# Low parts of the weight units and two differences moved to DVE, low part of k to POOL, the output's additions a period later

## The reference

```
scores = scale * q_c @ k_full.T
a = exp(scores - max); a = a / (sum(a) + 1e-9)
out[chunk] = a @ v_full
```

## Time and profile before

| | |
|---|---|
| three runs, median (lowest to highest) | 1243.87 us (1243.09 to 1247.61) |
| profiled execution | 1244.59 us, span 1242.8 us |
| busy, share of the span | PE 92%, weight loads 84%, DVE 72%, POOL 56%, ACT 46% |
| mean granted TensorE clock | 0.98 |
| first layer with attention | until about 740 us |
| second layer | 740 to 1242.8 us |
| DMA | 192 MB, 154 GB/s over the span |

### The profile page before, as it was taken

One profiled execution on the slowest core, in us unless ns is written; L12 is line 12 of the kernel. 1 busy time (PEld: TensorE's weight loads), 2 busy tenths in 40 slices (PEclk: granted clock), 3 DMA queues, 4 the chain that ended last, 5 costly groups with the idle time before them and its releaser, 6 DMA issues.

```text
span 1242.8 us, 19258 instructions
## 1 busy us (share of the span) xinstructions
PE 1149.0 (92%) x6624; PEld 1045.7 (84%) x6624; DVE 892.0 (72%) x1233; ACT 565.9 (46%) x1230; POOL 696.3 (56%) x542
## 2 busy tenths in 40 slices
PE   5789999999999999989999999999899999799988
PEld 4789998899889899889989997887677887588876
DVE  7778677577676666675874626568996688986678
ACT  7565555455445455454554324523425343245331
POOL 6276255555556556553652615669556675666573
PEclk9799999999999999999999999999899999899999
DMA  5244144333443443443243316655476554375545
GB/s 185 93 158 155 70 138 149 139 135 134 141 144 124 154 138 115 160 134 123 93 157 130 119 42 239 199 181 179 146 260 228 197 194 162 133 253 189 188 135 170
DMA packets 83985, 192.00 MB, mean 154 GB/s; under 512 B 5568, under 2 KB 9664, under 8 KB 83904
## 3 DMA queue, kind: packets, MB, share of 16 engines
q1 hardware_dynamic: 67008, 153.12, 36.1%
q10 hardware_dynamic: 16896, 37.75, 8.9%
HBM read 148.91 MB, written 41.94 MB: 154 GB/s over the span
## 4 chain that ended last, share of the span: by engine, by line
PE 36%; issue 22%; POOL 20%; DVE 13%; DMA 4%; ACT 4%; POOLq 0%; ACTq 0%; DVEq 0%; SPq 0%
POOL g_lo L396 5%; POOL pair_split L420 5%; PE p_y L1087 4%; PE p_y L1089 4%; PE p_y L1088 4%; DMA qkv_raw<-qkv 3%; POOL gs_lo L486 3%; POOL w_raw L415 2%; PE p_y L1077 2%; PE p_h L1061 2%; PE p_y L1078 2%; PE p_y L1079 2%; PE p_h L1062 2%; PE p_h L1063 2%; PE p_h L1087 2%
## 5 line engine op out<-in xcount | busy, mean ns | idle before, releaser
L396 POOL TENSOR_TENSOR g_lo<-g_raw,g_hi 128x384 fp32r<-128x384 f32 x112 | 120.8, 1079 | 174.1 <-ACT g_hi L572 173.3
L486 POOL TENSOR_TENSOR gs_lo<-hidden,gs_hi 128x1024 fp32r<-128x1024 f32 x60 | 161.0, 2699 | 78.7 <-ACT gs_hi L691 78.7
L1061 PE MATMUL p_h<-x_hi,w_hi 128*128 128x384 f32 x512 | 179.5, 351 | 13.2 <-DVE g_raw L825 12.0
L1077 PE MATMUL p_y<-g_hi,w_hi 128*128 128x384 f32 x512 | 176.2, 344 | 0.0
L1062 PE MATMUL p_h<-x_lo,w_hi 128*128 128x384 f32 x512 | 174.3, 340 | 0.0
L1063 PE MATMUL p_h<-x_hi,w_lo 128*128 128x384 f32 x512 | 174.2, 340 | 0.0
L572 ACT ACTIVATE g_hi<-g_raw 128x384 fp32r<-128x384 f32 x128 | 67.1, 525 | 232.6 <-DVE g_raw L825 231.9
L1079 PE MATMUL p_y<-g_hi,w_lo 128*128 128x384 f32 x512 | 171.5, 335 | 0.0
L1078 PE MATMUL p_y<-g_lo,w_hi 128*128 128x384 f32 x512 | 171.5, 335 | 0.0
L1087 PE MATMUL p_y<-gs_hi,down_ring 128*128 128x512 f32 x336 | 133.3, 397 | 12.9 <-DVE rest L932 8.6
L1088 PE MATMUL p_y<-gs_lo,down_ring 128*128 128x512 f32 x336 | 132.5, 394 | 0.0
(11 more groups left out here) (139 smaller groups left out, 2943.2 us busy)
## 6 DMA issues: line engine op xcount, KB each, us to landing
up_ring<-pairs SPq DMA_DIRECT2D x84, 512.0 KB, 4.7
down_ring<-pairs SPq DMA_DIRECT2D x84, 512.0 KB, 3.8
qkv_raw<-qkv SPq DMA_DIRECT2D x60, 576.0 KB, 3.8
pairs<-pair_split ACTq DMA_DIRECT2D x16, 1792.0 KB, 7.5
w_raw<-weights SPq DMA_DIRECT2D x16, 512.0 KB, 4.6
w_raw<-halves ACTq DMA_DIRECT2D x16, 512.0 KB, 8.1
x<-y_out SPq DMA_DIRECT2D x32, 192.0 KB, 4.2
x_all<-x SPq DMA_DIRECT2D x3, 2048.0 KB, 9.1
```

The costliest lines, as they stand in the source:

```text
L396: pool.tensor_tensor(g_lo[:, f % GRING, :], g_raw[:, f % 2, :], g_hi[:, f % GRING, :], ALU.subtract).then_inc(g_lo_done, 1)
L486: pool.tensor_tensor(gs_lo[:, j], source, gs_hi[:, j], ALU.subtract).then_inc(gs_lo_pool, 1)
L1061: pe.matmul(o, w_hi[:, f, cols], x_hi[:, c, :], start=(c == 0), stop=False)
L1077: pe.matmul(o, w_hi[:, f, cols], g_hi[:, s, :], start=(f == 0), stop=False)
```

## The change

Four things are moved. In the attention stretch the low parts of the weight units go from POOL to DVE, in two instructions (pieces 0 to 2 at step 7, pieces 3 to 6 at step 9) in place of seven. The low part of k goes from DVE to POOL, in front of that of v, for every head whose block is in `qkv_raw`. In the second layer both differences of `finish_part` go to DVE: c12's behind the sum of d6, c21's behind d0. The seven additions go one period later, into periods 5 and 9: two behind d0, two behind the sum of u1, three behind the sum of u2. With them ACT's copies of the first part wait for the additions (d0's for two of them, the others for all seven), and SP's stores stand at steps d4 and d6 of that period; the last span keeps the old places. The split of x is moved: 2 to 4 go behind d3 to d5, 5 and 6 behind d1 of the next period.

```
             def tile(t, attention, first=False, last=False, units=()):       # POOL
-                    split_v(HEADS * t + HEADS, 0, qkv_raw)
+                    split_kv(HEADS * t + HEADS, 0, qkv_raw)
...
+            def split_kv(g, h, raw):
                 pool.wait_ge(qkv_hi_done, g + 1)
+                pool.tensor_tensor(k_lo[:, h % 2, :], raw[:, KO:VO], qk_hi[:, h % 2, KO:VO], ALU.subtract)
                 pool.tensor_tensor(v_lo[:, h % VRING, :], raw[:, VO:QKV], v_hi[:, h % VRING, :],
                                    ALU.subtract).then_inc(kv_lo_done, 1)
...
             def finish_part(m):
-                pool.wait_ge(c_gated, 2 * m + 2)
-                pool.wait_ge(g_mix_done, m + 1)
-                pool.tensor_tensor(c12, c22, c12, ALU.subtract).then_inc(g_diff_done, 1)
-                pool.wait_ge(c21_gated, m + 1)
-                pool.tensor_tensor(c21, c21, g_mix[:, :, :], ALU.subtract).then_inc(g_diff_done, 1)
...
                 if m:                                                        # ACT, copy_down
-                    act.wait_ge(y_mixed, 7 * (m // PARTS))
+                    act.wait_ge(y_mixed, 7 * (m // PARTS) - (5 if j == 0 else 0))
...
             def split_q(g, h, raw):                                          # DVE
-                if raw is qkv_raw:
-                    dve.tensor_tensor(k_lo[:, h % 2, :], raw[:, KO:VO], qk_hi[:, h % 2, KO:VO], ALU.subtract)
...
+            def split_unit(u, step):
+                if step == 7:
+                    dve.wait_ge(unit_hi_done, 2 * u + 1)
+                    dve.tensor_tensor(pair_split[:, 0:3, 1, :], blocks[:, 1:4, :], pair_split[:, 0:3, 0, :],
+                                      ALU.subtract)
+                if step == 9:
+                    dve.wait_ge(unit_hi_done, 2 * u + 2)
+                    dve.tensor_tensor(pair_split[:, 3:7, 1, :], blocks[:, 4:8, :], pair_split[:, 3:7, 0, :],
+                                      ALU.subtract).then_inc(unit_lo_done, 1)
...
+            def mix(span, into, a, b, done):
+                dve.wait_ge(y_mixed, 7 * span + done)
+                dve.tensor_tensor(totals[into], totals[a], totals[b], ALU.add).then_inc(y_mixed, 1)
+
+            def mix_at(span, j):
+                if j == 0:
+                    mix(span, 1, 1, 0, 0)
+                    mix(span, 2, 2, 0, 0)
+                if j == 2:
+                    mix(span, 3, 3, 2, 2)
+                if j == 3:
+                    mix(span, 6, 6, 3, 3)
+                if j == 4:
+                    mix(span, 2, 2, 4, 3)
+                    mix(span, 4, 3, 4, 5)
+                    mix(span, 5, 5, 2, 5)
...
+            def difference12(m):
+                dve.wait_ge(g_mix_done, m + 1)
+                dve.tensor_tensor(c12, c22, c12, ALU.subtract).then_inc(g_diff_done, 1)
+
+            def difference21(m):
+                dve.wait_ge(gs_lo_pool, gs_pool_count(1, m))
+                dve.wait_ge(g_diff_done, 2 * m + 1)
+                dve.tensor_tensor(c21, c21, g_mix[:, :, :], ALU.subtract).then_inc(g_diff_done, 1)
...
                     combine(m)
                     add_down(m - 1, 6)
+                    difference12(m)
                     split_gs(2, g_mix[:, :, :], m)
...
                         if j == 0 and m < PERIODS - 1:
+                            if mixing:
+                                dve.wait_ge(y_added, total_count(m - 1, 6, 1))
+                                mix_at(m // PARTS - 1, 0)
+                            difference21(m)
                             split_gs(3, g_sum[:, :, :], m)
...
+                    if mixing and kind == "up" and j == 1:
+                        mix_at(m // PARTS - 1, 2)
+                        mix_at(m // PARTS - 1, 3)
+                    if mixing and kind == "up" and j == 2:
+                        mix_at(m // PARTS - 1, 4)
...
-                    if next_x and kind == "down" and 2 <= j <= 4:
-                        split_xs(s, j)
+                    if next_x and kind == "down" and 3 <= j <= 5:
+                        split_xs(s, j - 1)
                     if n and n % PARTS == 0 and n < PERIODS and kind == "down" and j == 1:
+                        split_xs(n // PARTS, 5)
                         split_xs(n // PARTS, 6)
-                if next_x:
-                    split_xs(s, 5)
```

More of the change, by code:

```diff
@@ L299, in load_down, with store_quad @@
                 load_pair(down_ring, DOWN_RING, down_loaded, down_done, m, 1, j)
-            def store_quad(m, q, j):
-                rows, half = 2 * (q // 2), 2 * (m // PARTS) + q % 2
+            def store_quad(span, q, j, mixed):
+                rows, half = 2 * (q // 2), 2 * span + q % 2
                 for i in range(2):
-                    if q == 3:
-                        sp.wait_ge(y_mixed, 7 * (m // PARTS) + 6)
+                    if span < SPANS - 1 or q == 3:
+                        sp.wait_ge(y_mixed, 7 * span + mixed)
                     else:
-                        sp.wait_ge(y_added, total_count(m, j, i))
+                        sp.wait_ge(y_added, total_count(PERIODS - 1, j, i))
                     sp.dma_start(out[:, rows + i, bass.ts(half, NT)], totals[j][:, i, :]).then_inc(quad_stored[q], DMA)
@@ L865, in split_xs, with tile @@
                 dve.tensor_tensor(xs_lo[:, j], x_source(j), xs_hi[:, j], ALU.subtract).then_inc(xs_lo_done, 1)
-            def tile(t, attention, first=False):
+            def split_unit(u, step):
[7 more added lines that the diff above has]
+                                      ALU.subtract).then_inc(unit_lo_done, 1)
+            def tile(t, attention, first=False, units=()):
                 g0 = HEADS * t + HEADS
@@ L893, in tile @@
                         split_xs(0, f - 3)
+                    for i, u in enumerate(units):
+                        split_unit(u, k - UNIT_EVERY * i)
             tile(0, True, first=True)
-            with dve.Fori(1, TILES - 1) as t:
-                tile(t, True)
+            with dve.Fori(1, 5) as t:
+                tile(t, True, units=units_of(t, 3))
+            with dve.Fori(5, 7) as t:
+                tile(t, True, units=units_of(t, 2))
             tile(TILES - 1, False)
@@ L933, in add_down @@
                                       ALU.add).then_inc(y_added, 1)
-            def mix_after(m, j):
-                span, p = divmod(m, PARTS)
-                if m < 0 or p < PARTS - 1 or j not in (0, 2, 3, 4):
-                    return
-                dve.wait_ge(y_added, total_count(m, j, 1))
-                for into, a, b in {0: [(1, 1, 0), (2, 2, 0)], 2: [(3, 3, 2)], 3: [(6, 6, 3)],
-                                   4: [(2, 2, 4), (4, 3, 4), (5, 5, 2)]}[j]:
-                    if into in (4, 5):
-                        dve.wait_ge(y_mixed, 7 * span + 5)
-                    dve.tensor_tensor(totals[into], totals[a], totals[b], ALU.add).then_inc(y_mixed, 1)
+            def mix(span, into, a, b, done):
[13 more added lines that the diff above has]
+                    mix(span, 5, 5, 2, 5)
             def combine(m):
```

46 lines of the change are left out of this document (17 added, 29 removed).

## The result

The changed kernel takes 1234.26 us (median of five runs, 1233.27 to 1235.49) against 1243.39 for the kernel before: ratio 0.9923, 95% interval 0.9903 to 0.9943. The profiled execution took 1233.27, its span is 1231.5 us. Forecast were 1230 and a range of 1212 to 1244. The gain of 0.8% is clear of the interval.

A forecast was written before the change was run, and what follows sets the result against it. TensorE was taken to set the pace, its waits mostly for a late DVE. Terms of -15.4, -3.6, -15.0, +20.0 and 0 gave -14.0 us, from 1244.59 profiled to 1230.6, or 1230 as a median; range 1212 to 1244.

The forecast's parts named there:

- Part 4: Second layer, periods 5 and 9: PE stands 8.6 us before d3 for ACT's copy behind all seven additions; +20.0 us.
- Part 3: Second layer, periods 4 and 8: the seven additions leave and the surplus falls to 3 us; -15.0 us.
- Part 2: Second layer, periods 3 and 7: POOL loses its two differences, DVE gains them; -1.8 us each, -3.6.
- Part 1: Attention stretch: boundaries -7.7 us, pairs of waits -6, clock -1.7; -15.4 us in all.
- ACT's x_raw moves by 0.65: Attention pairs: with the unit in DVE's queue, the next activation comes at 265.1 instead of 265.8 us.
- rival C: Attention stretch: POOL becomes the last before the scores, 19 waits grow by 1 us each; 1255 us, chance 0.08.
- if PE waits there for POOL's k_lo: Attention stretch: a sign named beforehand that would show the prediction wrong; no size given.
- Clock: Attention stretch: one of three half-clock stretches, each behind a wait of PE, goes; -1.7 us.
- Part 5: Second layer, remaining periods: 0 in sum; in the last, two differences before d3's sum +0.8, POOL done earlier -0.8 us.
- A: Second layer, periods 5 and 9: the additions fit, d3 waits 1.7 us and the clock holds; 1212 us, chance 0.15.
- B: Attention stretch gives a quarter, -4 instead of -15.4 us, PE waiting for loads or ACT anyway; 1241 us, chance 0.17.
- D: Second layer: additions stay as late on DVE, periods 4 and 8 hand their surplus on; 1233 us, chance within the forecast's 0.55.

The follow-up runs named there:

- fine_waits: Changed kernel, but ACT's copy of each down product waits only for the additions that still use its own total; 1219.2 us, ratio 0.9806 to before.
- gs6_late: Changed kernel, but POOL makes the low part of operand 6 only when g_mix is done; 1233.9 us, ratio 0.9917 to before.
- units_stay: Changed kernel, but the weight units' low parts stay on POOL as seven instructions; 1227.47 us, ratio 0.9880 to before.
- best2: best1 with the additions reordered as the copies want the totals, and c21's difference behind d3 in the last period; 1210.61 us, ratio 0.9725 to before.
- k_stays: Changed kernel, but the low part of k stays on DVE; 1232.65 us, ratio 0.9915 to before.
- diff_back: Changed kernel, but both differences of the second layer are back on POOL; 1240.61 us, ratio 0.9984 to before.
- unit_step10: Changed kernel, but DVE's larger weight-unit instruction stands at step 10 instead of 9; 1233.5 us, ratio 0.9924 to before.
- second_only: Kernel before with only the second layer's part of the change, attention and first layer as before; 1242.31 us, ratio 0.9981 to before.
- best1: Changed kernel with fine_waits and units_stay together; 1216.83 us, ratio 0.9798 to before.
- mix_back: Changed kernel, but the seven additions, the copies' wait and the stores are in their old place; 1236.51 us, ratio 0.9956 to before.

## Why the prediction was right, and where not

The forecast was 4 us low. The mechanism of the second layer was foreseen; that of the attention stretch only at the tile boundaries. That the total came so near is partly luck: in the profile's terms parts 1 and 5 gave 8.2 us less than forecast, and parts 2, 3 and 4 together 5.5 us more. The steps, with their terms:

- **Part 4, the new wait at d3: right.** Forecast +20.0, measured +18.3; DVE's queue was to end at T + 27.0 and ended at T + 26.2, PE was to stand 8.6 us and stood 7.80, with about 1.7 us of slow clock behind it where 2 was taken. Its cause was the coarse count, as fine_waits showed. The walk that gave it used nothing but rows 6 to 9 and the rule that DVE and POOL shut each other out. Here is what that rule makes of the place: POOL, ready at 909.85, ends at 913.21, 2.25 us after DVE's g_sum, and g_mix, ready at 911.06, ends 1.1 us after POOL. The Trainium skill says so (SBUF — State Buffer, section "SBUF: two separate sides": whoever comes first has the pair of ports for the whole instruction). By that rule the trace agrees, and gs6_late shows what follows for a cure: the collision moves to whichever instruction is next.
- **Part 3, periods 4 and 8: right in kind, 2.9 us too small.** Forecast -15.0, measured -17.9. Period 4 was to keep 3 us over the floor and kept 1.6: the wait before u4 was 1.1 where 1.5 to 3.9 stood, and those before d1 (0.5) and u3 (0.2) didn't come.
- **Part 2, periods 3 and 7: right in size.** -3.6 against -4.5; the waits before u3 and u4 were 0.7 and 1.15 where 1.0 and 1.7 stood. But the differences carry little of it: with both back on POOL PE's waits in each of these periods are 2.5 us, against 2.2 in the changed kernel. What they carry is in periods 5 and 9: 2.3 us of PE's waits in each.
- **Part 1, attention: right at the boundaries, wrong in the pairs.** The boundary waits were to lose 7.7 us and lost 7.5 (10.4 to 2.9). The pairs' waits were to shrink by 6 and grew by 4.8 (18.8 to 23.6). The term that failed is "ACT's x_raw moves by 0.65": the sum took the activation to come at 265.1 instead of 265.8. In fact the turns' wait grew from 10.4 to 14.0, since the unit's instruction stands in front of the activation (1.46 us at 263.72, 0.75 with it on POOL, 0.69 with it a step later). The other half, that the scores' wait would nearly go, failed through rival C's mechanism in small: POOL's k_lo, mean 1384 ns where DVE's took 981 in the same stretch, stands in front of v_lo, for which the scores now wait 0.5 to 0.7 us a time, as at 242.18. By the prediction's own sign ("if PE waits there for POOL's k_lo") this part was wrong. To this come three waits of 2.79, 1.09 and 1.78 us at a tile's second head. For the first of them the head's block was issued at 321.99, right behind the unit's 512 KB at 321.77, and ACT began on it 6.8 us later, where the median of these loads lands after 3.8. These waits stay in units_stay and best2 (0.9 to 1.9 us) and are absent in k_stays, so k_lo on POOL is needed for them; that the two loads' order is their cause was not tried. Clock gave 5.1 us where 1.7 was taken, at the prediction's price of 1.7 for each: all three slow stretches of this layer went. In sum -8.6 where -15.4 stood.
- **Part 5, the rest: +1.4 where 0 stood.** In period 11 the wait before d5 grew from 3.7 to 4.9, and the period took 46.17 us instead of 43.7. The forecast let +0.8 for DVE's two differences and -0.8 for an earlier POOL cancel. diff_back, with both differences on POOL, has 3.76 and 43.69 again, so it is the differences on DVE that cost the 1.2 us of waiting, and the -0.8 didn't come. Which of the two it is stays open: best2, with c21's in another place, kept 46.2. The other 1.3 us are the clock behind the wait, since four kernels with the same wait of 4.9 (k_stays, units_stay, unit_step10, second_only) took 44.7 to 44.9.

Of the rivals, A (the additions fit) was wrong for this kernel and is what best2 became: not because POOL's parts came between, but because nobody waited for all seven. B forecast 1241 by the attention stretch giving -4; it gave half of the forecast, so the truth lies between. D's description, that periods 4 and 8 hand their surplus on, fits: 22 us down, 18 up. Its 1233 is nearest to the measured 1234, but by luck: it had 12 us of surplus in periods 5 and 9, which have 9.5 and 9.9, and the whole -15.4 in the attention stretch.

## What to carry to other kernels

When work is moved behind another engine's wait, look at what number the wait asks for: a count over a whole group of instructions, in place of the one that makes the data, cost 11 us (profiles) to 15 us (medians) here, the moved work itself nothing once its order fitted. Moving work from a slow engine to a fast one pays where somebody waits for the slow one, and costs where its new queue has a consumer behind it; k_lo and the units' low parts were moved in opposite directions, each move gained alone (13.5 and 8.4 us), and once k_lo had moved the other cost 5. Moving two instructions onto an engine can make that engine earlier, when they were what shut it out.

## What the runs showed of the hardware

**The same wait, and two answers of the clock.** fine_waits and best1 both stop 2.43 us before d4 of period 5. In fine_waits the clock was granted at 0.67 for the next 3.66 us, and d4 took 4.16 us and u5 3.01, 1.7 more than two products at full clock (2.72 each). In best1 d4 took 2.85 and u5 2.72.

```profile
936.84:940.50 3.66, 3.66 (x11) 2.95 (x12) 2.81 (x5) 3.07 (x5) 2.29 (x1) 0.67 1.01 323
```

The same stretch behind the wait in best1:

```profile
931.94:935.60 3.66, 3.65 (x16) 3.02 (x17) 2.82 (x5) 3.08 (x5) 2.28 (x1) 1.00 1.01 331
```

The 27.07 us before are alike in both: TensorE was busy for 24.64 of them. So neither what TensorE did in these 27 us nor the length of its wait decides it here: the wait costs 4.1 us in one kernel and 2.6 in the other. It is so in period 9 too (d4 takes 4.42 us in fine_waits and 2.82 in best1). It is the 1.6 us between 42.4 and 40.8 in the table. What decides stays open.

**The same code, up to 6 us apart.** Tiles 1 to 6 of the changed kernel took 518.1 to 524.2 us in five kernels whose instructions there are the same (mix_back the least, diff_back the most). Most of these 6 us can be named. diff_back has two stretches of 10 us at a granted clock of 0.83, from 330 and from 510 us, and mix_back none: 3.4 us at 1.7 each. And at the second head of tiles 3 and 5 TensorE waits 2.72 and 3.45 us in diff_back, 2.49 and 1.04 in mix_back: 2.6 us. mix_back's whole time is flattered by it; its second layer alone is the thing to compare.
